# Four gate parts in another order: a kernel of linear attention, Fourier mixing and two feed-forward stages

## What is computed

```python
# 1. linear attention with a complex decay, per batch and head
mag = sqrt(a_re**2 + a_im**2)
scale = minimum(mag, 0.999) / (mag + 1e-6)        # |gate| is capped at 0.999
for t in range(S):                                 # S = 768
    S_re, S_im = ar*S_re - ai*S_im + k[t] v[t]^T,  ar*S_im + ai*S_re
    y[t] = q[t] @ S_re
# 2. Fourier mixing and a feed-forward layer
u = x + real(fft(fft(x, axis=1), axis=2))          # 768 tokens x 384 channels
u = u + relu(layernorm(u) @ w_ch1) @ w_ch2         # 384 -> 1536 -> 384
# 3. token mixing (w_tok1, w_tok2) and a second channel layer of the same size
```

## Time and profile before

| | |
|---|---|
| runs | 1060.64, 1064.76, 1067.88 us |
| profiled execution | 1054.72 us, span 1052.7 us |
| TensorE busy | 987.1 us (94%) |
| VectorE busy | 514.6 us |
| ScalarE busy | 357.9 us |
| attention and transforms | 0 to about 379 us |
| channel stages | from there to 1045 us |

### The profile page before, as it was taken

One profiled execution on the slowest core, in us unless ns is written; L12 is line 12 of the kernel. 1 busy time (PEld: TensorE's weight loads), 2 busy tenths in 40 slices (PEclk: granted clock), 3 DMA queues, 4 the chain that ended last, 5 costly groups with the idle time before them and its releaser, 6 DMA issues.

```text
span 1052.7 us, 15640 instructions
## 1 busy us (share of the span) xinstructions
PE 987.1 (94%) x6154; PEld 947.3 (90%) x6154; DVE 514.6 (49%) x980; ACT 357.9 (34%) x532; POOL 16.4 (2%) x12
## 2 busy tenths in 40 slices
PE   0389999999999999999999999999999999999997
PEld 0268889889899899999999999999999999999997
DVE  5888799999946654324234322542323314223220
ACT  7676666676621510220220221431203102121220
POOL 0000000000000000000000000030000000000000
PEclk9789899999999999999999999999999999999999
DMA  6689977986785056021021020010001001000000
GB/s 207 196 233 246 263 227 185 228 260 145 187 238 205 16 192 221 16 75 45 15 75 45 22 68 23 16 53 16 8 24 45 22 15 52 22 0 22 9 16 25
DMA packets 96602, 104.68 MB, mean 99 GB/s; under 512 B 13089, under 2 KB 90145, under 8 KB 96546
## 3 DMA queue, kind: packets, MB, share of 16 engines
q1 hardware_dynamic: 96546, 103.94, 33.8%
HBM read 70.80 MB, written 33.11 MB: 99 GB/s over the span
## 4 chain that ended last, share of the span: by engine, by line
PE 77%; DVE 12%; ACT 7%; issue 2%; DMA 0%; SPq 0%; DVEq 0%; ACTq 0%
PE bank L232 21%; PE bank L233 21%; PE bank L234 21%; DVE n_area L932 3%; PE bank L1162 2%; PE bank L1223 2%; PE bank L1180 2%; PE bank L1239 2%; PE bank L242 1%; PE bank L1178 1%; PE bank L1241 1%; DVE n_area L937 1%; PE bank L1191 1%; PE bank L1247 1%; DVE n_area L920 1%
## 5 line engine op out<-in xcount | busy, mean ns | idle before, releaser
L120 ACT ACTIVATE hh<-bank 128x384 fp32r<-128x384 f32 x192 | 94.5, 492 | 377.1 <-PE bank L234 377.1
L208 DVE SCALAR_TENSOR_TENSOR hl<-bank,hh 128x384 fp32r<-128x384 f32 x192 | 107.1, 558 | 195.5 <-ACT hh L120 195.5
L232 PE MATMUL bank<-w2h,hh 128*128 128x384 f32 x576 | 193.2, 335 | 0.0
L232 PE MATMUL bank<-nTh,w1h 128*128 128x384 f32 x576 | 193.0, 335 | 0.0
L234 PE MATMUL bank<-w2h,hl 128*128 128x384 f32 x576 | 192.5, 334 | 0.0
L234 PE MATMUL bank<-nTh,w1l 128*128 128x384 f32 x576 | 192.5, 334 | 0.0
L233 PE MATMUL bank<-nTl,w1h 128*128 128x384 f32 x576 | 192.4, 334 | 0.0
L233 PE MATMUL bank<-w2l,hh 128*128 128x384 f32 x576 | 192.4, 334 | 0.0
L232 PEld LDWEIGHTS bank<-nTh,w1h 128*128 128x128 f32 x576 | 108.1, 188 | 0.4 <-issue 0.3
L233 PEld LDWEIGHTS bank<-w2l,hh 128*128 128x128 f32 x576 | 108.2, 188 | 0.0
L232 PEld LDWEIGHTS bank<-w2h,hh 128*128 128x128 f32 x576 | 108.1, 188 | 0.0
(11 more groups left out here) (153 smaller groups left out, 1292.4 us busy)
## 6 DMA issues: line engine op xcount, KB each, us to landing
w_area<-k_turn SPq DMA_DIRECT2D x24, 384.0 KB, 4.6
w_area<-q_turn SPq DMA_DIRECT2D x24, 384.0 KB, 6.0
q_turn<-w_raw SPq DMA_DIRECT2D x30, 192.0 KB, 2.8
k_turn<-n_area SPq DMA_DIRECT2D x24, 192.0 KB, 2.5
k_turn<-w_flat SPq DMA_DIRECT2D x24, 192.0 KB, 2.7
u_scratch<-h_area SPq DMA_DIRECT2D x24, 192.0 KB, 6.4
w_raw<-in_moe_w_ch SPq DMA_DIRECT2D x2, 2304.0 KB, 13.0
x_flat<-u_scratch SPq DMA_DIRECT2D x4, 1152.0 KB, 10.3
```

Source lines behind the costliest of these rows:

```text
L120: self.nc.scalar.activation(self.hh[:, m, :], self.mm_bank[(g * (KF + TPG) + m) % 2][:, 0:TG], ACT.Relu).then_inc(self.h_high, 1)
L208: self.nc.vector.scalar_tensor_tensor(out=self.hl[:, m, :], in0=self.mm_bank[(g * (KF + TPG) + m) % 2][:, 0:TG], scalar=0.0, in1=self.hh[: ...
L232: self.nc.tensor.matmul(out, lh, rh, start=(n == 0), stop=False)
```

## The change

The change edits the attention alone.

1. **Order of the first parts.** ScalarE's and VectorE's lists for p0 to p3 and chunks 0 to 2 are written out. The loop starts at m = 3. `logs` is cut into `bounded` and `sums`. `factors`, `sums`, `ends` and `scaled` get semaphores of their own (`factored`, `summed`, `ended`, `qk_scaled`), so that they can stand at another place than the count gave them.
2. **One scan a part.** `sums` sets the first element of every chunk to -1e30 and puts its old value in the floor, so that one scan of 1152 columns restarts at each chunk by itself. The floor is now 1152 columns wide. For p0 and p1 there is one scan for each group of channels.
3. **Alternating term.** The table of +1 and -1 in `sequence_transform` becomes 128 rows x 128 columns, all but the first row zero, instead of 1 x 768; its other operand `a_mid` gets 128 rows, all but the first zero.
4. **Fewer matmuls of zeros.** Chunks 0 to 5 have 12, 3, 6, 2, 2 and 4 of them instead of 5 each. The 8 of chunks 6, 12 and 18 are gone.
5. SyncE's list for the first chunks has another order: `turn_out(0)`, `turn_back(0)`, the gates of p3, and only then p1. Its `decay_out(p2)` at m = 0 stays where it was.

```diff
-        GA = 16
-        GV = [10 + 3 * p.chunks + 2 * len(PAIRS[p.n]) for p in parts]
+        GA = 14
+        GV = [6 + 3 * p.chunks + 2 * len(PAIRS[p.n]) for p in parts]
...
-        alt = tok_raw[0:1, 2 * 3 * TM:2 * 3 * TM + S]
+        alt = tok_raw[:, 2 * 3 * TM:2 * 3 * TM + P]
...
+        factored, summed, ended, qk_scaled = (sems(x, 2) for x in ("factored", "summed", "ended", "qk_scaled"))
...
             decay_out(p0)
+            turn_out(0)
+            turn_back(0)
+            decay_back(p0)
+            load_gates(p3)
             decay_out(p1)
-            turn_out(0)
-            decay_back(p0)
-            decay_back(p1)
-            turn_back(0)
             turn_out(1)
             turn_out(2)
-            load_gates(p3)
+            decay_back(p1)
             turn_back(1)
             turn_back(2)
...
             squares(p0)
+            magnitudes(p0)
             squares(p1)
-            magnitudes(p0)
+            inverses(p0)
             magnitudes(p1)
-            inverses(p0)
             factors(p0)
             inverses(p1)
-            factors(p1)
             angle_tables()
             arctangents(p0)
             arctangents(p1)
             sines(p0)
             squares(p2)
+            logarithm_tables()
+            factors(p1)
+            magnitudes(p2)
+            angle_tables()
             sines(p1)
+            keys_turned(0)
             logarithm_tables()
-            magnitudes(p2)
             inverses(p2)
+            angle_tables()
+            arctangents(p2)
+            logarithm_tables()
             factors(p2)
+            keys_turned(1)
+            squares(p3)
             angle_tables()
-            for m in range(NM):
+            evacuate_y(0)
+            sines(p2)
+            y_turned(0)
+            keys_turned(2)
+            logarithm_tables()
+            magnitudes(p3)
+            inverses(p3)
+            factors(p3)
+            evacuate_y(1)
+            angle_tables()
+            y_turned(1)
+            for m in range(3, NM):
...
-                for g, i in product(range(3), range(p.chunks)):
-                    log = t1_b[s][:, g, i * CT:(i + 1) * CT]
-                    last = V.tensor_tensor_scan(log, log, bottom[:, :], 0.0, ALU.add, ALU.max)
-                last.then_inc(vec_step[s], 1)
+                V.tensor_scalar(floors[:, ::CT].rearrange("p (g c) -> p g c", g=3), starts, LOG_FLOOR, None, ALU.max).then_inc(restarts_set, 1)
+                dve.wait_ge(restarts_set, 2 * p.n + 1)
+                V.memset(starts, CUT).then_inc(restarts_set, 1)
+                dve.wait_ge(restarts_set, 2 * p.n + 2)
+                for line, floor in lines:
+                    last = V.tensor_tensor_scan(line, line, floor, 0.0, ALU.add, ALU.max)
+                last.then_inc(summed[s], 1)
...
             squared(p0)
+            bounded(p0)
+            dve.wait_ge(consts_set, 5)
+            sums(p0)
             squared(p1)
-            dve.wait_ge(consts_set, 5)
-            logs(p0)
-            logs(p1)
+            tangents(p0)
+            bounded(p1)
+            sums(p1)
+            tangents(p1)
             ends(p0)
-            tangents(p0)
             scaled(p0)
+            phases(p0)
+            products(p0, PAIRS[0])
+            squared(p2)
+            phases(p1)
             ends(p1)
-            tangents(p1)
-            phases(p0)
             scaled(p1)
-            products(p0, PAIRS[0])
-            phases(p1)
-            squared(p2)
+            bounded(p2)
             products(p1, PAIRS[1])
-            logs(p2)
+            tangents(p2)
+            sums(p2)
+            dve.wait_ge(tables_in, 2 * 16)
+            masked(0)
+            advance_state(0)
+            phases(p2)
             ends(p2)
-            tangents(p2)
             scaled(p2)
-            dve.wait_ge(tables_in, 2 * 16)
-            for m in range(NM):
+            products(p2, PAIRS[2][0:1])
+            masked(1)
+            squared(p3)
+            products(p2, PAIRS[2][1:2])
+            advance_state(1)
+            bounded(p3)
+            masked(2)
+            sums(p3)
+            ends(p3)
+            tangents(p3)
+            scaled(p3)
+            for m in range(3, NM):
...
-                mm(out[:, 0:FH], alt[:, rows], a_mid[:, :], start=True, stop=False)
+                mm(out[:, 0:FH], alt, a_mid[:, :], start=True, stop=False)
...
+            WARM = [12, 3, 6, 2, 2, 4]
...
-                    keep_busy(5)
+                    keep_busy(WARM[m])
...
-                if b and j == 0:
-                    if b > 1:
-                        pe.wait_ge(b_added, (b - 1) * NT - 1)
-                    keep_busy(8)
```

More of the change, by code:

```diff
@@ L37 @@
 LOG_FLOOR = -84.0
+CUT = -1e30
 END_FLOOR = 4.248354255291589e-18
@@ L481, in products_done @@
         def products_done(p, i):
-            return vec0[p.n] + 10 + 3 * p.chunks + 2 * (i // 2)
+            return vec0[p.n] + 6 + 3 * p.chunks + 2 * (i // 2)
         def angles_room(p):
@@ L703, in magnitudes @@
                 for o in parts[max(p.n - 2, 0):p.n] if p.n > 1 else []:
-                    act.wait_ge(vec_step[o.s], vec0[o.n] + 7 + 3 * o.chunks)
+                    act.wait_ge(vec_step[o.s], vec0[o.n] + 3 + 3 * o.chunks)
                 A(t4[:, :, angles_room(p)], re_b[p.r][:, :, T], ACT.Abs).then_inc(act_step[s], 1)
@@ L733, in sines @@
                 re, im = re_b[p.r], im_b[p.r]
-                act.wait_ge(vec_step[s], vec0[p.n] + 9 + 3 * p.chunks)
+                act.wait_ge(vec_step[s], vec0[p.n] + 5 + 3 * p.chunks)
                 A(re[:, :, T], t3_b[s][:, :, T], ACT.Abs).then_inc(act_step[s], 1)
                 A(im[:, :, T], t3_b[s][:, :, T], ACT.Sin, scale=TURN).then_inc(act_step[s], 1)
-                act.wait_ge(act_step[s], n + 14)
+                act.wait_ge(act_step[s], n + 12)
                 A(re[:, :, T], re[:, :, T], ACT.Sin, scale=-TURN, bias=half_pi[:, 0:1]).then_inc(act_step[s], 1)
@@ L776, in _ @@
             logarithm_tables()
-            p0, p1, p2 = parts[0:3]
+            p0, p1, p2, p3 = parts[0:4]
             squares(p0)
+            magnitudes(p0)
             squares(p1)
-            magnitudes(p0)
+            inverses(p0)
             magnitudes(p1)
-            inverses(p0)
             factors(p0)
             inverses(p1)
-            factors(p1)
             angle_tables()
@@ L886, in logs, with sums @@
                 V.tensor_tensor(t3_b[s][:, :, T], t3_b[s][:, :, T], t4[:, :, angles_room(p)], ALU.add).then_inc(vec_step[s], 1)
-                dve.wait_ge(vec_step[s], n + 2)
-                for g, i in product(range(3), range(p.chunks)):
-                    log = t1_b[s][:, g, i * CT:(i + 1) * CT]
-                    last = V.tensor_tensor_scan(log, log, bottom[:, :], 0.0, ALU.add, ALU.max)
-                last.then_inc(vec_step[s], 1)
+            def sums(p):
+                s, T = p.s, slice(0, p.T)
+                dve.wait_ge(vec_step[s], vec0[p.n] + 2)
+                starts, floors = t1_b[s][:, :, 0:p.T:CT], bottom[:, 0:3 * p.T]
+                if p.T == TM:
+                    lines = [(t1_b[s].rearrange("p g t -> p (g t)"), floors)]
+                else:
+                    lines = [(t1_b[s][:, g, T], floors[:, g * p.T:(g + 1) * p.T]) for g in range(3)]
+                V.tensor_scalar(floors[:, ::CT].rearrange("p (g c) -> p g c", g=3), starts, LOG_FLOOR, None, ALU.max).then_inc(restarts_set, 1)
[5 more added lines that the diff above has]
+                last.then_inc(summed[s], 1)
             def ends(p):
                 s = p.s
-                dve.wait_ge(act_step[s], act0[p.n] + 9)
-                V.tensor_copy(dstage[:, p.n, :, 0:p.chunks], t2_b[s][:, :, CT - 1:p.T:CT]).then_inc(vec_step[s], 1)
+                dve.wait_ge(factored[s], 2 * p.turn + 1)
+                V.tensor_copy(dstage[:, p.n, :, 0:p.chunks], t2_b[s][:, :, CT - 1:p.T:CT]).then_inc(ended[s], 1)
             def tangents(p):
-                s, T, n = p.s, slice(0, p.T), vec0[p.n]
-                re, im = re_b[p.r], im_b[p.r]
+                s, T = p.s, slice(0, p.T)
+                im = im_b[p.r]
                 dve.wait_ge(act_step[s], act0[p.n] + 8)
@@ L943, in products @@
                 re, im = re_b[p.r], im_b[p.r]
-                dve.wait_ge(act_step[s], act0[p.n] + 16)
+                dve.wait_ge(act_step[s], act0[p.n] + 14)
+                dve.wait_ge(qk_scaled[s], 2 * (p.turn + 1))
                 for pair in chunks:
@@ L1005, in add_transform @@
                 V.tensor_tensor(high, high, sn[:, 1:FH - 1], ALU.add).then_inc(b_added, 1)
-            V.memset(s0.power, -0.5).then_inc(s0.power_set, 1)
             V.memset(half_pi[:, :], PI / 2).then_inc(consts_set, 1)
@@ L1054, in _ @@
                 if m == NM - 2:
+                    V.memset(s0.power, -0.5).then_inc(s0.power_set, 1)
                     s0.moments_of(dve, 0, first=True)
@@ L1058, in _ @@
                 if (m, 1) in stage_at:
```

(5 more changed lines are left out.)

58 lines of the change are left out of this document (29 added, 29 removed).

## The result

| | before | after |
|---|---|---|
| median of 20 runs | 1061.79 us | 1067.76 us |
| lowest and highest | 1052.98, 1070.26 | 1060.75, 1071.22 |
| profiled span | 1052.7 us | 1065.7 us |
| granted clock of it | 0.982 | 0.944 |

The ratio of the two is 1.0064, with a 95% interval of 1.0043 to 1.0086. It compares means and leaves out runs more than 1.5% above the fastest of their kernel, here two of before. I give differences as ratios times 1060 us: 6.8 us slower here (the medians differ by 6.0), within the 1% that I called no change. I had forecast 14.8 us. The profiled pair differs by 13.0 us, because the profiled run of before was one of its better ones; its own runs spread over 17 us, and the experiments show why.

A forecast was written before the change was run, and what follows sets the result against it. TensorE was taken to carry 77% of the chain, with gains and losses arising in the attention. The sum 2.5 + 15 - 2.7 = +14.8 us on a median of 1064.8 gave 1080 us, 8-in-10 range 1052 to 1089.

The forecast's parts named there:

- reordering and counts of zeros: Chunks 0 to 5: new order and new zero matmul counts bring the copy of y 2.5 us later.
- one scan: VectorE's single scan of 1152 columns for nine: 0 us, -0.2 to +0.3 a part.
- alternating term: Sequence transforms: 128 rows cost 0.18 us less, 24 times, about 15 of them counting: -2.7 us, bounds 0 and -4.3.
- crossings: Chunks 6, 12 and 18 without zero matmuls: clock falls, next chunk at half clock, 5 us each, +15 us, bounds 0 and 18.
- the opening: Everything ahead of p4's arctangents, chunks 0 to 5: copy of y 2.5 us later.
- Reordering up to p2: p2's arctangents at about 43.3 us, phases 47.9, products about 60; chunk 1's outputs at about 65 instead of 75.35.
- Chunks 1 and 2: Chunk 2 at half clock, 10.3 instead of 5.39 us; p3's arctangents 1.6 us earlier, 5.7 at full clock.
- Chunks 3 to 5: Chunk 4 entered at half clock, chunk 5's zero matmuls partly at full; copy of y 2.5 us later.
- The baseline: +14.8 us on the profiled 1054.7 us gives 1069.5; on an expected median of 1064.8 it gives 1080.
- the first two rivals: Clock holds in chunks 2 to 5, batches pay: 1070, chance 0.13; chunk 7's scores bring the clock back: 1069, chance 0.16.
- The third rival: ScalarE's new order decides, the clock does not; pauses of chunks 6, 12, 18 stay hidden: 1053 us, chance 0.26.

The follow-up runs named there:

- o_only: Changed kernel with the one-row alternating term, nine scans, five zero matmuls in each of chunks 0 to 5, eight at crossings; 1059.2 us, 1.0001 of before.
- a_nine: Changed kernel with nine scans, five zero matmuls in each of chunks 0 to 5 and the eight at the crossings; 1048.6 us, 0.9883 of before.
- a_keep8_five: Changed kernel with five zero matmuls in each of chunks 0 to 5 and the eight of chunks 6, 12 and 18 back; 1049.95 us, 0.9925 of before.
- a_keep8: Changed kernel with only the eight zero matmuls of chunks 6, 12 and 18 put back; 1049.7 us, 0.9921 of before.
- c_fill: a_keep8 plus 5 zero matmuls ahead of chunk 1's outputs and 4 ahead of chunk 3's; 1051.5 us, 0.9917 of before.
- b_look3: The kernel before, unchanged, profiled again; 1059.2 us.
- a_tan8: a_keep8 with VectorE's tangents of chunks 11 and 17 ahead of its products and masks instead of behind; 1059.3 us, 0.9997 of before.
- b_look2: The kernel before, unchanged, profiled again; 1055.5 us.
- b_look: The kernel before, unchanged, profiled again; 1050.5 us.

## Why the prediction was wrong, by its own steps

The single changes add up from before to after (o_only, a_nine, a_keep8_five, a_keep8, after), in ratios times 1060 us:

| part | forecast | measured |
|---|---|---|
| reordering and counts of zeros | +2.5 | 0 and -0.4 |
| one scan | 0 | +4.9, not told from 0 |
| alternating term | -2.7 | -12.9 |
| crossings | +15 | +15.2 |
| sum | +14.8 | +6.8 |

The step that failed is the term for the alternating matmul, -2.7 us in the sum and -12.9 measured (point 5). Next to it the opening, +2.5 us, was worth nothing (point 3).

1. **Reordering up to p2: right.** 43.3, 47.9, 60 and 65 us were forecast; 44.19, 48.76, 60.52 and 65.45 came. The table changes cost 1.28 us and the next activation starts 1.30 us after the start of one (47.80 to 49.10; after the one ahead of p2's arctangents 1.41), as in the earlier trace rows; the further drain that the Trainium skill, "ScalarE: Activation LUTs", section "What ACT_TABLE_LOAD costs", states is not in this trace either.
2. **Chunks 1 and 2: right.** The outputs of chunk 1 and all of chunk 2 ran at half clock, as I put it (62.3 to 82.8 us), and the arctangents of p3 came 0.9 us earlier (85.40 against 86.27), forecast 1.6. The 5.7 that I gave for the full clock does not follow from my terms, which would make about 11; c_fill ran there at the full clock, and its copy of y ahead of these arctangents came 5.5 us earlier than before (80.36 against 85.88).
3. **Chunks 3 to 5: wrong by 4.3 us in the profiled pair.** I let chunk 5 run partly at half clock and the copy of y come 2.5 us later, at 126; it came 1.85 earlier, at 122.09. The clock rose at 113.5 us, 3.1 us after the two matmuls of zeros of chunk 4 began (110.40), as it had risen 3.3 us into the five before (109.58 to 112.9). I took it that two don't last that long; they lasted 2.89 us, the clock rose in the transposes of y right behind them, and chunk 5 ran at the full clock. By ratios the whole reordering is worth nothing: o_only's ratio is 1.
4. **The crossings: right in mechanism and size.** The pause was 4.50 us (forecast 4.5), the clock fell 2.6 us into the first, at 134.0, and against a_keep8 the copies of y lost 4.4, 4.4 and 5.5 us (forecast 5 each). What I had not forecast is a further fall at 314.9 us, 4.9 us more, in a chunk without a pause. In the kernel before, the same zeros are worth 26.8 us: 17.3 at the crossings of the profiled pair, and 8.1 at a fall outside them.
5. **The alternating term: the step that failed.** I took 0.18 us per transform from the step into the next group alone, which was to shrink to 0.34. It shrank by 0.12, to 0.40, but the edge ahead of the term (0.09) and the one behind the next group (0.10) are shorter too: 0.31 in these rows, 0.35 between copies of y. About 14 transforms count; I had 15. That makes 4.9 us where I had 2.7. The other 8.0 us go by falls of the clock, which the reordered kernel has more often with the one-row term than with the 128-row one. The cause of that stays open, and in the kernel before the term is worth 3.9 us in all. I had no place for this in the sum: I treated falls as something that pauses cause at fixed places, while the earlier trace rows is one draw of several.
6. **The baseline.** Against its own profiled execution the forecast was 1069.5 us, and the profiled execution of after took 1067.7. I carried the whole difference over to the median, but the median run of before, 7 us longer, probably holds one or two falls more than the profiled one already: the median granted clock of its runs in the later sets is 0.975 to 0.978, where the profiled run has 0.982, and b_look3 with two falls has 0.975 and 1059.2 us. The changed kernel's profiled run is a median one by its time. So the pair of profiles flattered the forecast, by luck: in it the opening (4.3 us better than forecast) and the fall at 314.9 us (4.9 worse) nearly cancel.

The measured 1067.8 us lies nearest to the first two rivals, 1070 and 1069, but neither happened. The clock did not hold in chunks 2 to 5, and in chunk 7 the scores did not bring it back: it rose at 147.6 us, behind the update. The third rival (no cost at the crossings, 1053 us) is near what a_keep8 gives, 1049.7, where the zeros hold the clock; its reason was another, since without the zeros the crossings did cost.

## What to carry to other kernels

Matmuls of zeros in a wait look free to remove, since something else ends the wait; what they hold up is the clock of the chunk behind it, and that is priced at the slower level over that whole chunk: 4.4 to 5.5 us at each of three crossings here. Where runs of one kernel differ by more than the effect that is looked for, list the falls of the clock in several profiles before taking one as the baseline. Moving one step forward does not help if its engine is busy throughout (a_tan8), and filling a pause can make it turn up one chunk later (c_fill). A gain of 4.4 us in one stage, as c_fill had, can be lost to a single later fall, so follow a gain along the whole stage before calling the change useless.

## What was not expected of the hardware

- A stretch with no wait over 0.30 us lost the clock (314.9 us in the changed kernel, 174.4 us in b_look2), while b_look, the same program as b_look2, kept it there. In the 3 us ahead of each fall TensorE did short matmuls, of 48 to 128 columns. The Trainium skill, "TensorE: Matmul & The Clock Gate", section "A second HAM failure mode: psum-queue depth-cycling", describes a kernel whose clock goes back and forth because TensorE is briefly idle between groups of matmuls. These traces agree in that no long wait is needed; that brief idle times are the cause here no run shows.
- A matmul with one row of weights between 128-row neighbours costs more than its 128-row form. The weight load takes 183 ns with one row and 190 with 128, so it hardly gets shorter with fewer rows, and yet the matmul itself takes 360 and 327 ns (medians), and a whole transform (update's start to the transposes) 3.99 and 3.68 us.
- One scan of 1152 columns takes 2.56 us where nine of 128 took 2.94, but the two small steps and their waits give it back.
